# Attention on one core: the short chunk of the scores first, the second head's minimum in one instruction, and the products with v in seven visits

## The reference

```python
q_pool = q.reshape(B, H, S // 2, 2, D).mean(axis=3)      # 1152 rows of q become 576
scores = scale * np.matmul(q_pool, k.transpose(0, 1, 3, 2))   # 576 x 1152 for each head
scores = scores - np.max(scores, axis=-1, keepdims=True)
attn = np.exp(scores)
attn = attn / (np.sum(attn, axis=-1, keepdims=True) + 1e-09)
return np.matmul(attn, v)                                # 576 x 64 for each head
```

## Time and profile before

| | us |
|---|---|
| median of three runs | 919.76 |
| the profiled execution | 917.36 |
| its span in the trace | 915.6 |
| TensorE busy | 817.7 (89%) |
| VectorE busy | 551.7 (60%) |
| ScalarE busy | 487.3 (53%) |
| TensorE's granted clock, mean of the span | 0.988 |

### The profile page before, as it was taken

One profiled execution on the slowest core, in us unless ns is written; L12 is line 12 of the kernel. 1 busy time (PEld: TensorE's weight loads), 2 busy tenths in 40 slices (PEclk: granted clock), 3 DMA queues, 4 the chain that ended last, 5 costly groups with the idle time before them and its releaser, 6 DMA issues. The chain is left out here.

```text
span 915.6 us, 16591 instructions
## 1 busy us (share of the span) xinstructions
PE 817.7 (89%) x5819; PEld 595.7 (65%) x5819; DVE 551.7 (60%) x1112; ACT 487.3 (53%) x729; POOL 248.7 (27%) x154
## 2 busy tenths in 40 slices
PE   4899899899899898898899898878578999999998
PEld 3666666666666666666666666544235888888886
DVE  3666666666766666667667666350007667766673
ACT  2555565555555555555655654321019666666662
POOL 2304304304214124124034030000008544443333
PEclk9999999999999999999999999989989999999999
DMA  5343203213113023023023061707990000000000
GB/s 129 140 126 78 61 20 78 48 30 77 30 48 77 15 63 77 1 76 77 0 77 78 1 236 67 276 2 291 395 401 15 24 24 23 23 23 23 23 22 24
DMA packets 82161, 75.50 MB, mean 82 GB/s; under 512 B 42448, under 2 KB 60880, under 8 KB 81616
## 3 DMA queue, kind: packets, MB, share of 16 engines
q1 hardware_dynamic: 79792, 74.47, 25.6%
q10 hardware_dynamic: 2336, 0.59, 0.3%
HBM read 70.32 MB, written 4.72 MB: 82 GB/s over the span
## 5 line engine op out<-in xcount | busy, mean ns | idle before, releaser
L478 ACT ACTIVATE prob<-ps,neg_max 128x1152 f32<-128x1152 f32 x144 | 175.8, 1221 | 213.4 <-DVE spare L395 213.4
L280 PE MATMUL ps<-ident,prob 128*128 128x128 f32 x1296 | 174.6, 281 | 51.4 <-ACT prob L478 49.9
L391 DVE TENSOR_REDUCE part_neg<-ps 128x1 f32<-128x512 f32 x288 | 191.8, 688 | 46.2 <-PE ps L254 37.3
L280 PEld LDWEIGHTS ps<-ident,prob 128*128 128x128 f32 x1296 | 140.8, 142 | 107.0 <-ACT prob L478 97.9
L296 PE MATMUL ps<-probT,v_nat 128*64 128x256 f32 (+1 forms) x1152 | 160.5, 414 | 0.0
L363 DVE COPY probT<-ps 128x128 f32<-128x128 f32 (+1 forms) x192 | 75.5, 421 | 101.9 <-PE ps L280 101.9
L451 ACT ACTIVATE probT<-ps 128x512 f32<-128x512 f32 x208 | 116.8, 593 | 33.8 <-PE ps L280 33.8
L208 POOL TENSOR_TENSOR kT<-k_raw,ones 128x1152 fp32r<-128x1152 f32 x15 | 31.6, 2107 | 342.4 <-DVE k_raw L432 342.4
L254 PE MATMUL ps<-kT,qT_hi 64*128 64x512 f32 (+1 forms) x768 | 111.7, 366 | 4.8 <-DVE qT_lo L380 2.6
L296 PEld LDWEIGHTS ps<-probT,v_nat 128*64 128x64 f32 x1152 | 74.5, 136 | 51.2 <-issue 10.9
L948 PE MATMUL ps<-w_hi,g_even 128*128 128x512 f32 x320 | 102.7, 392 | 2.2 <-POOL g_even L1032 2.0
(11 more groups left out here) (142 smaller groups left out, 1002.9 us busy)
## 6 DMA issues: line engine op xcount, KB each, us to landing
slot<-in_moe_w SPq DMA_DIRECT2D x16, 2048.0 KB, 12.8
v_nat<-in_v SPq DMA_DIRECT2D x16, 576.0 KB, 4.8
k_nat<-in_k SPq DMA_DIRECT2D x30, 288.0 KB, 4.0
q_nat<-in_q SPq DMA_DIRECT2D x32, 256.0 KB, 4.2
out<-res SPq DMA_DIRECT2D x18, 256.0 KB, 2.0
slot<-in_moe_w_in SPq DMA_DIRECT2D x2, 2048.0 KB, 20.7
slot<-in_moe_w_out SPq DMA_DIRECT2D x8, 512.0 KB, 16.8
q_nat_r<-in_q SPq DMA_DIRECT2D x32, 32.0 KB, 3.6
```

What stands on the lines that cost most here:

```text
L280: last = nc.tensor.transpose(dst[:, n * P:(n + 1) * P], prob[h][:, kt * P:(kt + 1) * P], ident[:])
L391: nc.vector.tensor_reduce(part[:, c:c + 1], ps[:, 3 * h + c, :], AX.X, ALU.min).then_inc(part_done, 1)
L478: nc.scalar.activation(prob[h][:], row, ACT.Exp, bias=neg_max[:, j:j + 1], scale=-1.0, accum_out=sums).then_inc(exp_done, 1)
```

## The change

- The chunks of the scores come in the order 2, 0, 1 (SCORE_ORDER): the short one first.
- VectorE reduces chunk 2 of both heads and chunk 0 of head 0. Head 0's tensor_scalar now runs over chunk 1 (512 columns). Head 1's runs over chunks 0 and 1 in one instruction (1024 columns) and takes chunk 2's part with it.
- The transposed chunks of head 1 lie in banks 6, 4, 3 in place of 6, 5, 4, and banks_free waits accordingly: chunk 2 waits for the copy of head 0's chunk 2 (third_evac), chunk 0 for the first evacuation and, other than in the mixed round and the one after it, for head 1's third_evac, chunk 1 for second_a and second_b. In round 3 chunk 2 also waits for q_evac.
- In the mixed round ScalarE copies q ahead of the evacuation of chunk 0, not behind it.
- The products with v go from six entries to seven: 8 + 4 in round 0 (10 + 2 before), 6 in round 1 as before, 8 + 2 in round 3 as before, 6 + 2 in round 4 (8 before).
- SyncE waits for neg_done instead of scores_full before one late load of weights, and some tiles get other addresses.

```diff
-    PV_AT = {(3, 0): (0, 0, 0, 8), (3, 1): (0, 0, 8, 10), (4, 0): (0, 0, 10, 18),
-             (0, 0): (1, 1, 0, 10), (0, 1): (1, 1, 10, 12), (1, 0): (1, 1, 12, 18)}
+    PV_AT = {(3, 0): (0, 0, 0, 8), (3, 1): (0, 0, 8, 10), (4, 0): (0, 0, 10, 16), (4, 1): (0, 0, 16, 18),
+             (0, 0): (1, 1, 0, 8), (0, 1): (1, 1, 8, 12), (1, 0): (1, 1, 12, 18)}
+    SCORE_ORDER = (2, 0, 1)
...
-            return ps[:, (c, (TBANK, 5, 4)[c])[h], 0:n]
+            return ps[:, (c, (TBANK, 4, 3)[c])[h], 0:n]
...
-            def banks_free(p, r, c, first, last):
-
-                before = tiles_of(p, r)
-                if c == 0:
-                    wait(pe, first_evac, before - (0 if r == MIX + 1 else 1))
+            def banks_free(p, r, c, last):
+
+                done = tiles_of(p, r)
+                firsts = done - (0 if r == MIX + 1 else 1)
+                if c == 2:
+                    wait(pe, third_evac, firsts)
+                    if r == MIX + 1 and not last:
+                        pe.wait_ge(q_evac, p + 1)
+                elif c == 0:
+                    wait(pe, first_evac, firsts)
                     if r == MIX + 1 and not last:
                         pe.wait_ge(k_copied, p + 1)
-                elif c == 1:
+                    elif r != MIX:
+                        wait(pe, third_evac, done)
+                else:
                     wait(pe, second_a, p * ROUNDS + r)
-                    wait(pe, third_evac, before)
-                elif r == MIX + 1 and not last:
-                    pe.wait_ge(q_evac, p + 1)
-                elif r != MIX:
-                    wait(pe, second_b, doubles_of(p, r))
+                    if r != MIX:
+                        wait(pe, second_b, doubles_of(p, r))
...
-            def maximum(p, r, h):
+            def small(p, r, h, c, slot):
+
+                dve.wait_ge(scores_full, (p * ROUNDS + r) * NCH + SCORE_ORDER.index(c) + 1)
+                nc.vector.tensor_reduce(part_neg[:, h, slot:slot + 1], ps[:, 3 * h + c, 0:(CHUNK[c][1] - CHUNK[c][0]) * P],
+                                        AX.X, ALU.min).then_inc(part_done, 1)
+
+            def smallest(p, r, h, c0, c1, parts, slot):
...
+                dve.wait_ge(scores_full, (p * ROUNDS + r) * NCH + NCH)
+                dve.wait_ge(part_done, parts)
                 wait(dve, exp_done, tau - TILES + 1)
-                nc.vector.tensor_scalar(spare[:], ps[:, 3 * h + 2, 0:P], part[:, 0:1], part[:, 1:2],
+                row = flat[:, (3 * h + c0) * BANK:(3 * h + c1) * BANK]
+                nc.vector.tensor_scalar(spare[h][:], row, part_neg[:, h, 0:1], part_neg[:, h, slot:slot + 1],
                                         ALU.min, ALU.min, accum_out=neg_max[:, j:j + 1]).then_inc(neg_done, 1)
+
+            def minima(p, r):
+
+                wait(dve, neg_done, tiles_of(p, r))
+                parts = p * (3 * ROUNDS - 1) + 3 * r - (1 if r > MIX else 0)
+                for h in range(heads_of(r)):
+                    small(p, r, h, 2, 0)
+                small(p, r, 0, 0, 1)
+                smallest(p, r, 0, 1, 2, parts + heads_of(r) + 1, 1)
+                if r != MIX:
+                    smallest(p, r, 1, 0, 2, parts + heads_of(r) + 1, 0)
...
+                    if r == MIX and not last:
+                        act.wait_ge(qtr_full, p + 2)
+                        act.wait_ge(k_copied, p + 1)
+                        wait(act, q_low, p)
+                        nc.scalar.activation(q_raw[:], q_row, ACT.Copy, scale=EXP_SCALE).then_inc(q_evac, 1)
                     group_free(act, p, r)
                     act.wait_ge(ptr_full, tau * NCH + 1)
                     evac(copy, r, 0, 0).then_inc(first_evac, 1)
```

More of the change, by code:

```diff
@@ L79, in attention @@
         part_neg = sb("part_neg", [P, 2, 2])
-        spare = sb("spare", [P, P])
+        spare = [sb(f"spare{h}", [P, (h + 1) * BANK]) for h in range(2)]
         neg_max = sb("neg_max", [P, TILES])
@@ L315, in body @@
                 for r in range(ROUNDS):
-                    for c in range(NCH):
-                        banks_free(p, r, c, first, last)
-                        if r == 0 and c == 0:
+                    for c in SCORE_ORDER:
+                        banks_free(p, r, c, last)
+                        if r == 0 and c == SCORE_ORDER[0]:
                             if first:
@@ L328, in body @@
                         wait(pe, second_b, doubles_of(p, r))
+                        wait(pe, third_evac, tiles_of(p, r))
                         turn_q_rest(p + 1, ps[:, TBANK - 1, BANK - P:BANK])
@@ L422, in body @@
                     tau = tiles_of(p, r)
-                    for h in range(heads_of(r)):
-                        maximum(p, r, h)
+                    minima(p, r)
                     if r == 0 and not first:
```

27 lines of the change are left out of this document (6 added, 21 removed).

## The result

The changed kernel takes 956.8 us (median of 4 runs, 953.3 to 959.3) against 919.7 for the kernel before (4 runs, 917.1 to 921.6): a ratio of 1.040, interval 1.036 to 1.044. It is slower, as predicted, but by 37 us where 16 were forecast, and 956.8 lies beyond the range of 926 to 946.

The account below looks back on a forecast made before the run. TensorE's own queue or the VectorE-ScalarE chain ends each round. Rounds 1, 0, 4, 3 and mixed (-0.35+0.57+0.30-0.13+0.68) make 1.07 a pair, 16.2 with the first pair's extra, so 936.0 us; range 926 to 946.

Parts of the forecast that it names:

- What bounds the kernel: Ahead of a set of transposes, either the VectorE-ScalarE chain or TensorE's queue ends last; TensorE busy 89% at 2.4 GHz.
- Part 1, the minima: Round 1, from its scores' start S: head 0's exponential at S+3.20, 0.14 later; head 1's at S+4.47, 0.35 earlier.
- the second pass: Rival: tensor_scalar passes each column twice, costing 0.37 more over 512, 0.87 over 1024; 988 us; chance 0.04.
- the double rate: Rival: tensor_scalar reads PSUM at 0.52 ns a column; +2 us, 922; chance 0.04.
- a hold of 0.06: Start of a round's scores: chunk 0, waiting for VectorE's copy of head 1's chunk 2, is held 0.06.
- the same +0.14 for every round: Head 0's exponential, and the transposes behind it, come 0.14 later, worked out in round 1 and used for rounds 0 and 4.
- Part 2, the visits: Products between the two heads' transposes hold head 1's; with the 0.14, round 0 +0.57 and round 4 +0.30.
- faster: Rival: added products in rounds 0 and 4 run in the transposes' shadow; -0.72 a pair, 908.3 us; chance 0.06.
- Part 2, the mixed round: Mixed round into round 3: first chunk waits for third_evac, +0.79; with an exponential 0.11 earlier, +0.68 is left.
- the wait is hidden: Rival: the mixed round's wait is hidden as copies end sooner or the chunk goes ahead; +3.6, 923.4 us; chance 0.05.

Follow-up runs that it names:

- One instruction alone: Kernel before, with only head 1's minimum over its first 1024 columns taken by one instruction; 906.8 us, ratio 0.987.
- Wait alone: Kernel before, with round 3's first chunk of scores also waiting for the copy of the mixed tile's last chunk (third_evac); 934.9 us, ratio 1.017.
- no wait: Changed kernel, with the mixed tile's transposed chunk 2 in bank 7, so round 3's first chunk has no new wait; 935.3 us, ratio 1.019.
- short copy first: Changed kernel, with VectorE copying chunk 2 ahead of chunk 1 in the mixed round; 942.1 us, ratio 1.025.
- no wait, old visits: Changed kernel, with the mixed tile's transposed chunk 2 in bank 7 and the old table of visits; 917.4 us, ratio 0.999.
- and five visits: Kernel before, with head 1's one-instruction minimum and the two products between round 0's transposes moved to round 1; 904.6 us, ratio 0.982.
- visits alone: Kernel before, with only the changed table of visits (8 + 4 products in round 0, 6 + 2 in round 4); 927.5 us, ratio 1.009.

## Why the prediction was right, and where it went wrong

**What bounds the kernel** was read rightly: a full round ends with whichever is later, VectorE and ScalarE's chain or TensorE's own queue; edits on one side are lost to the other. "One instruction alone" shows it at its plainest: head 1's exponential comes earlier in every full round, and rounds 1 and 4 get 0.48 and 0.28 shorter, rounds 0 and 3 not at all.

**Part 1, the minima.** The tensor_scalar's price was right at both sizes (0.81 and 1.34, forecast 0.81 and 1.35). This settles the rivals "the second pass" and "the double rate": 1024 columns take 0.53 more than 512, 1.04 ns a column, one pass at the rate of the reduces. By the line of the Trainium skill, "VectorE: DVE Perf Modes", section on the perf-mode tier table, that allows a tensor_scalar up to 2x from any PSUM operand, they could have been shorter; these rows go with the line of its subsection "Why PSUM operands drop a tier", that float32 from PSUM has 1x.

**The failed step in part 1: "That gives S+0.51 for the load and some 0.04 more for the matmul, against a natural S+0.49: a hold of 0.06."** The start was right: chunk 0 starts at S+0.54. The natural time wasn't: without the hold chunk 0 starts at S+0.39. And behind the wait its matmuls are slower to get going, which no term had. So the hold was 0.22 instead of 0.06, in rounds 0, 1 and 4, and my lower and upper ends (nothing to 0.17 in three rounds) didn't hold it. A second error hides a part of this one: without a hold chunk 0 is full at S+1.34, where I had 1.38. Together they make the reduce 0.12 late in three rounds, 0.36 of the 0.82 that the pair was missed by. The tensor_scalar's start, 0.20 behind the reduce instead of 0.14 in round 1, is another 0.18 if it is the same in all three.

**A further step, smaller: the same +0.14 for every round.** It was worked out in round 1 and laid on rounds 0 and 4 as well. In round 4 head 0's transposes come at S+4.74, 0.42 behind the S+4.32 of before, while in round 1 the exponential moved by 0.33. And in the mixed round, where the forecast has the exponential 0.11 earlier, the transposes come 0.07 later (S+4.57, 333.31 to 337.88, against S+4.50). Each round's chain had to be followed on its own.

**Part 2, the visits**: right. Alone they cost 0.60 a pair. Round 0 is 0.44 longer in that kernel (301.42 to 309.19, 7.77) and round 4 0.17 (7.28); the forecast's 0.57 and 0.30 are, without the 0.14 that part 1 adds to each, 0.43 and 0.16. With it the rival "faster" falls: nothing of the products runs in the shadow of the transposes. The visits cost 0.97 in the changed kernel because in round 4 they no longer fill idle time; the forecast had that in its sum, which lets the products hold head 1's transposes 0.64 beyond its exponential there.

**Part 2, the mixed round**: the wait is there and has nearly the size that was forecast (2.08 from the transposes, forecast 2.1). By itself it costs 0.65 a pair, the 0.78 of the mixed round less the 0.13 of round 3, as in the sum (0.79 and 0.13). Taken out of the changed kernel it is worth 0.89 to 0.91, since there the short chunk can then start right behind the transposes. The rival "the wait is hidden" falls.

**The failed step that cost most: the wait of the mixed round was priced at the clock of the kernel before.** "TensorE is busy 89% of the span at a clock that stands at its upper level (2.4 GHz) in all of attention, so what it idles there is small and what it is given to do counts" held for the old kernel only. The wait lengthens a stretch of transposes and idle time from 3.90 to 4.69 us, and behind it TensorE runs round 3's scores at 1.2 GHz in some of the pairs: +1.5 each. With the first and last pairs the lower clock is about a third of the profiled difference, and it is in no term or rival of mine. "Wait alone" brings it to round 3 in the loop with nothing else changed; "no wait" ends it there; "short copy first" shortens the stretch and nearly ends it. What the experiments tie to the wait are the six slow rounds 3 between the first pair and the last, 9 of the 13.5 us; the first and the last pair lose their clock in kernels without the wait too. The Trainium skill, "TensorE: Matmul & The Clock Gate", Part 4 on the PE-mode transpose, says that a transpose doesn't count as busy for the gate in the same way as other matmuls. If it doesn't count at all, the stretch is all idle, and that should have been a rival of this prediction. The runs go with it as far as they go: products in the stretch end the lower clock of round 3 inside the loop. But the rule alone doesn't say why the old 3.90 never brought it there, or why with 4.69 only some pairs are long.

**The range** was too narrow, and mostly for the clock. With chunk 0 full when it was (0.36 a pair) the forecast would have been 16.2 + 0.36 x 15 = 21.6, or 941, within the range. With all of the short pair's 1.87 it would have been 28 and 948, 2 us above the range; the clock took it the rest of the way to 957.

**What stays open:** which pairs are long. They aren't every other one, and DMA share doesn't tell them apart. Open too is the lower clock in the first pair and in the last. In the first pair's round 1 the short chunk's place isn't the cause by itself: "no wait, old visits" has it in front and keeps the upper clock there, "and five visits" has it behind and loses it.

## What to carry to other kernels

A wait put in front of a whole stage can cost more than its length where TensorE had only transposes and idle time before it: read the granted clock by windows there, and ask what the engine did since its last real matmul. Reordering chunks so that a short one comes first can move a wait that was hidden behind the first chunk onto the path; follow each wait to its new place, and give a wait in the middle of a run of matmuls more than its length (here 0.22 for a stop of 0.15). Work that is moved to fill one gap opens another, and the clock can fall there. And try the parts of a change alone: here one instruction of it was worth 13 us, and the edits around it cost 50, the lower clock included.

## What the runs showed of the hardware that was not expected

- After 4.69 us of transposes and idle time TensorE ran the next scores at a granted clock of 0.51, in some pairs and not in others; after 3.90 us in the same place it never did. The scores took 3.48 instead of 1.92, and the clock was back at once behind them. With eight rows of products inside the stretch, round 3 kept the upper clock in all fourteen pairs between the first and the last.
- The length of such a stretch doesn't decide alone: in the last pair, where 2.46 us of it are idle in one piece, the clock fell in "visits alone" and kept its upper level in the kernel before, after 3.77 us in all.
- A kernel whose pairs all do the same work has pairs of two lengths, 36.93 and 38.5. A mean over pairs, or the page's 40 slices, hide it.
- A stop between two chunks of scores of 0.15 us delays the reader of the chunk behind it by 0.22.
- tensor_scalar with two pointer scalars and an accumulator, float32 from PSUM: 0.41, 0.81 and 1.34 us for 128, 512 and 1024 columns.
